# Two heads per keys-times-values matmul in a chunked recurrence with two feed-forward blocks, fp32, one core

## The reference, cut to what matters

```python
# q, k, v, o_gate: [4, 8, 768, 40]; i_gate, f_gate: [4, 8, 768]
for t in range(S):
    m_new = max(f[t] + m, i[t])
    f_stab, i_stab = exp(f[t] + m - m_new), exp(i[t] - m_new);  m = m_new
    C = f_stab * C + i_stab * outer(v[t], k[t])          # 40 x 40 state per head
    n = f_stab * n + i_stab * k[t]
    y[t] = sigmoid(o[t]) * (C @ q[t]) / max(abs(n . q[t]), 1)
x  = y.reshape(3072, 320)
x1 = ((x @ w1) * (x @ w2)) @ w3 @ w_out                   # 320 -> 1024 -> 1024 -> 320
y  = max(x1 @ u1, x1 @ u2, x1 @ u3) @ u_out               # 320 -> 768 -> 320
```

## Time and profile before

| | us |
|---|---|
| median of 3 runs | 710.59 (709.71 to 710.85) |
| profiled execution | 705.52 |
| its span | 703.6 |
| PE busy | 687.3 (98%) |
| PE weight loads busy | 574.5 (82%) |
| DVE busy | 448.6 (64%) |
| ACT busy | 290.5 (41%) |
| POOL busy | 126.1 (18%) |

### The profile page before, as it was taken

The page is one execution under the profiler, slowest core; times in us unless marked ns, Lnnn a source line. Parts: engine busy times, 40 slices in busy tenths (PEclk is TensorE's granted clock), DMA queues, the critical chain, the costliest instruction groups (busy, mean ns, idle before and its releaser), DMA issues.

```text
span 703.6 us, 11573 instructions
## 1 busy us (share of the span) xinstructions
PE 687.3 (98%) x3662; PEld 574.5 (82%) x3662; DVE 448.6 (64%) x819; ACT 290.5 (41%) x640; POOL 126.1 (18%) x153
## 2 busy tenths in 40 slices
PE   5999999999999999999999999999999999999997
PEld 4886888788888888888888888888888888888785
DVE  6678898854688853687853588863578873322423
ACT  1645756333645322654422555422645522322211
POOL 4232434000334100232200143200133200000000
PEclk9999999999999999999999999999999999999999
DMA  8897376060454400355400244510154100100001
GB/s 274 276 270 200 114 202 168 27 146 21 129 134 116 119 25 0 99 140 135 118 24 0 89 122 121 152 33 0 50 153 117 58 0 0 37 1 1 0 1 37
DMA packets 69311, 65.27 MB, mean 93 GB/s; under 512 B 29972, under 2 KB 47700, under 8 KB 69284
## 3 DMA queue, kind: packets, MB, share of 16 engines
q1 hardware_dynamic: 69284, 64.92, 33.3%
HBM read 58.72 MB, written 4.03 MB: 89 GB/s over the span
## 4 chain that ended last, share of the span: by engine, by line
PE 88%; DVE 3%; DMA 3%; issue 2%; SPq 1%; ACT 1%; POOL 0%; POOLq 0%
PE ring L448 52%; PE acc L448 22%; PE ybank L448 9%; PE sbank L448 3%; DMA og_s<-in_og 3%; PE tbank L448 1%; PE tbank L535 1%; DMA w1o_raw<-in_wout 1%; DVE gate L890 1%; ACT gm L655 1%; DVE sc_s L841 0%; DVE hid L911 0%; DVE q_st L851 0%; POOL decay_s L409 0%; DVE x1T L1009 0%
## 5 line engine op out<-in xcount | busy, mean ns | idle before, releaser
L448 PE MATMUL ring<-x1T,mx_hi 128*128 128x512 f32 x432 | 152.5, 393 | 0.1
L448 PE MATMUL ring<-xT,ab_hi 128*128 128x512 f32 x384 | 136.6, 396 | 0.0
L655 ACT ACTIVATE gm<-hid 128x512 fp32r<-128x512 f32 x84 | 53.1, 632 | 164.9 <-DVE hid L923 131.2
L409 POOL TENSOR_TENSOR decay_s<-decay_s,causal 128x512 f32<-128x512 f32 x48 | 63.2, 1317 | 205.3 <-DMA og_s<-in_og 197.9
L448 PE MATMUL acc<-gm,wp 128*128 128x512 f32 x384 | 97.4, 395 | 0.4 <-DVE gm L904 0.4
L448 PEld LDWEIGHTS ring<-x1T,mx_hi 128*128 128x128 f32 x432 | 81.2, 188 | 17.6 <-issue 0.5
L904 DVE TENSOR_TENSOR gm<-hid,gm 128x512 fp32r<-128x512 f32 x84 | 58.2, 692 | 54.2 <-ACT gm L655 54.2
L655 ACT ACTIVATE left<-ring 128x512 f32<-128x512 f32 x84 | 49.9, 594 | 87.5 <-PE ring L448 87.5
L448 PEld LDWEIGHTS acc<-gm,wp 128*128 128x128 f32 x384 | 71.6, 188 | 16.9 <-ACT gm L655 0.8
L448 PE MATMUL ring<-x1T,mx_lo 128*128 128x512 f32 x216 | 84.1, 389 | 0.0
L448 PEld LDWEIGHTS ring<-xT,ab_hi 128*128 128x128 f32 x384 | 72.2, 188 | 14.4 <-ACT xT L655 0.2
(11 more groups left out here) (130 smaller groups left out, 1020.0 us busy)
## 6 DMA issues: line engine op xcount, KB each, us to landing
decay_s<-phi_d SPq DMA_DIRECT2D x48, 256.0 KB
k_s<-in_kT SPq DMA_DIRECT2D x40, 240.0 KB
q_s<-in_qT SPq DMA_DIRECT2D x40, 240.0 KB
w_raw<-in_w3T SPq DMA_DIRECT2D x8, 512.0 KB, 4.5
kn_s<-in_kn SPq DMA_DIRECT2D x48, 80.0 KB
og_s<-in_og SPq DMA_DIRECT2D x48, 80.0 KB
vn_s<-in_vn SPq DMA_DIRECT2D x48, 80.0 KB, 2.4
out_y<-stage SPq DMA_DIRECT2D x12, 256.0 KB, 2.1
```

Source lines behind the costliest of these rows:

```text
L409: pool.tensor_tensor(d4, d4, causal[:].unsqueeze(1).broadcast_to([P, HQ, L]), ALU.add).then_inc(s["masked"], 1)
L448: return pe.matmul(o, l, r, start=start, stop=stop)
L655: return act.activation(o, i, ACT.Copy)
```

## The change

The keys-times-values product of a quad is done in two matmuls, one for each pair of heads: 80 stationary columns (`kw_s` of both heads) and 84 moving ones (`vn_s` of both heads). Of the 80 x 84 result only the two blocks on the diagonal mean something: rows 0 to 39 with the first head's 42 columns, rows 40 to 79 with the second's. The state takes this layout, `state[80, side, quad, pair, 42]`, the blocks off the diagonal included, and `ybank` is written so that a side's pairs lie together. VectorE fades and adds in one scalar_tensor_tensor for each pair, with a factor for each of the 80 rows. These factors are the exponentials of the chunk-end sums, all made once: the sums go out to `last_d` and come back to `last_s` over 40 rows twice (two small loads), ScalarE makes `fades`, and VectorE copies a chunk's 16 columns to `fade_now` and the `since` factors to `since_now` once in each body (`chunk_factors`). GpSimd's fades and ScalarE's small exponentials go.

High and low parts of the state are written to `c_part` (over xT's memory; for chunk 0 `c_first`, over x1T's), and six DMAs of 40 rows bring the diagonal blocks to `c_st`. For the last chunk there is no keys-times-values product, no weighing of keys, no load of `kn_s`, no fade and no stacking; so body 4 is written out too, and the loop covers bodies 1 to 3. Two orders shift: the pieces of `beside1` behind its fourth place go one iteration earlier, and weight piece 6 is loaded behind quad 7 of the opening, not ahead of it.

```diff
             def stack_state(c):
                 sp.wait_ge(s["c_lo"], c + 1)
-                sp.dma_start(c_st[DIM:2 * DIM].bitcast(F32), state[LOW:LOW + DIM]).then_inc(s["c_in"], 16)
-                sp.dma_start(c_st[2 * DIM:ST].bitcast(F32), c_st[0:DIM].bitcast(F32)).then_inc(s["c_in"], 16)
+                parts = c_parts(c)
+                for r, part in enumerate((0, 1, 0)):
+                    for side in range(2):
+                        sp.dma_start(f32(c_st[r * DIM:(r + 1) * DIM, side]).rearrange("p k j d -> p (k j d)"),
+                                     f32(parts[side * DIM:(side + 1) * DIM, part, side * (CW // 2):(side + 1) * (CW // 2)])
+                                     ).then_inc(s["c_in"], 16)
...
-                load_piece(k)
-            load_piece(QUADS)
+                    sp.dma_start(last_d, g_phi[:].rearrange("b (c t) -> b c t", t=L)[:, :, L - 1],
+                                 allow_slow_non_contiguous=True).then_inc(s["last_out"], 16)
+                if k == 4:
+                    sp.wait_ge(s["last_out"], 16)
+                    for side in range(2):
+                        sp.dma_start(last_s[side * DIM:(side + 1) * DIM],
+                                     last_d.rearrange("(j s) c -> s j c", s=2)[side].partition_broadcast(DIM)
+                                     ).then_inc(s["fades_in"], 16)
+                if k < N_AB:
+                    load_piece(k)
+            for n in range(N_AB, N_AB + NSTAGE):
+                load_piece(n)
...
                 for h in range(HQ):
                     hs, hd = slice(h * L, (h + 1) * L), slice(h * DN, (h + 1) * DN)
-                    mm(ybank[:, hd], sc_s[:, slot, hs], vn_s[:, slot, h, :], True, True)
+                    last = mm(ybank[:, hd], sc_s[:, slot, hs], vn_s[:, slot, h, :], True, True)
                     if not first:
-                        mm(ybank[:, HQ * DN + h * DN:HQ * DN + (h + 1) * DN], q_st[:, slot, hs], c_st[:, k, hd], True, True)
-                    last = mm(ybank[0:SQ, 2 * HQ * DN + h * DN:2 * HQ * DN + (h + 1) * DN],
-                              kw_s[:, slot, h * DIM:h * DIM + SQ], vn_s[:, slot, h, :], True, True)
+                        last = mm(ybank[:, HQ * DN + h * DN:HQ * DN + (h + 1) * DN], q_st[:, slot, hs],
+                                  c_st[:, h % 2, k, h // 2, :], True, True)
+                if not final(c):
+                    for j in range(PAIRS):
+                        last = mm(across(ybank[0:PAIR, 2 * HQ * DN:3 * HQ * DN])[:, :, j, :],
+                                  kw_s[:, slot, j * PAIR:(j + 1) * PAIR], vn_s[:, slot, 2 * j:2 * j + 2, :], True, True)
...
             def x_hi(c, u):
                 act.wait_ge(s["turned"], 3 * c + u + 1)
+                if u == 0 and not (isinstance(c, int) and c in (0, CHUNKS - 1)):
+                    act.wait_ge(s["c_in"], 16 * C_LOADS * (c + 1))
...
-                dve.wait_ge(s["faded_ok"], n - QUADS + 1)
-                dve.tensor_tensor(state[0:DIM, k, :], ybank[0:DIM, 2 * HQ * DN:3 * HQ * DN], faded[:, slot, :], ALU.add)
+                if not final(c):
+                    for j in range(PAIRS):
+                        mine = state[:, :, k, j, :]
+                        dve.scalar_tensor_tensor(out=mine, in0=mine, scalar=fade_now[:, k * PAIRS + j:k * PAIRS + j + 1],
+                                                 in1=across(ybank[0:PAIR, 2 * HQ * DN:3 * HQ * DN])[:, :, j, :],
+                                                 op0=ALU.mult, op1=ALU.add)
...
-        beside1 = [[], [N_AB, N_AB + 1], [N_AB + 2], [N_AB + 3], [], [N_AB + 4], [N_AB + 5], [N_AB + 6]]
+        beside1 = [[], [N_AB, N_AB + 1], [N_AB + 2], [N_AB + 3], [N_AB + 4], [N_AB + 5], [N_AB + 6], []]
```

More of the change, by code:

```diff
@@ L103, in build @@
         sc_s = sb("sc_s", [P, 2, HQ * L])
[L104 to L108, removed]
+        kw_s = sb("kw_s", [P, 2, HQ * DIM])
+        state = sb("state", [PAIR, 2, QUADS, PAIRS, DN])
+        c_st = sb("c_st", [ST, 2, QUADS, PAIRS, DN], F32R)
+        last_s = sb("last_s", [PAIR, QUADS * PAIRS, CHUNKS])
+        fades = sb("fades", [PAIR, CHUNKS, QUADS * PAIRS])
+        fade_now = sb("fade_now", [PAIR, QUADS * PAIRS])
+        since_now = sb("since_now", [P, BH])
         heads = sb("heads", [P, HQ, DN])
@@ L222, in quad, with final, quad_loaded, c_parts @@
             return c * QUADS + k
+        def final(c):
+            return isinstance(c, int) and c == CHUNKS - 1
+        def quad_loaded(c, k):
+            if final(c):
+                return 16 * (LOADS * c * (QUADS // 2) + (LOADS - 1) * (k // 2 + 1))
+            return 16 * LOADS * (c * (QUADS // 2) + k // 2 + 1)
+        def c_parts(c):
+            return c_first if isinstance(c, int) and c == 0 else c_part
+        def across(pairs):
+            return pairs.rearrange("p (s j d) -> p s j d", j=PAIRS, d=DN)
         def split(n):
@@ L368, in _ @@
             body(0, False)
-            with sp.Fori(1, CHUNKS - 1) as c:
+            with sp.Fori(1, CHUNKS - 2) as c:
                 body(c, True)
+            body(CHUNKS - 2, True)
             store_group(CHUNKS - 2)
@@ L414, in weigh_keys @@
                 w4 = gcol[:, c, 2 * BH + k * HQ:2 * BH + (k + 1) * HQ].unsqueeze(2).broadcast_to([P, HQ, DIM])
-                pool.tensor_tensor(kw_s[:, slot, 0:HQ * DIM].rearrange("p (h e) -> p h e", e=DIM),
+                pool.tensor_tensor(kw_s[:, slot, :].rearrange("p (h e) -> p h e", e=DIM),
                                    kn_s[:, slot, :].rearrange("p (h e) -> p h e", e=DIM), w4, ALU.mult).then_inc(s["kw_ok"], 1)
[L418 to L430, removed]
-                    fade_state(c, k)
-                    if k + 1 < QUADS:
-                        mask(c, k + 1)
-                        weigh_keys(c, k + 1)
             pool.wait_ge(s["gcol_ok"], 2)
@@ L440, in _ @@
             pool.wait_ge(s["gcol_rest"], 2)
-            with pool.Fori(1, CHUNKS) as c:
-                body(c)
+            with pool.Fori(1, CHUNKS - 1) as c:
+                for k in range(QUADS):
+                    mask(c, k)
+                    weigh_keys(c, k)
+            for k in range(QUADS):
+                mask(CHUNKS - 1, k)
         @block.tensor
@@ L646, in _ @@
             body(0, True)
-            with pe.Fori(1, CHUNKS - 1) as c:
+            with pe.Fori(1, CHUNKS - 2) as c:
                 body(c, True)
+            body(CHUNKS - 2, True)
             body(CHUNKS - 1, False)
@@ L700, in c_hi @@
                 act.wait_ge(s["evacuated"], QUADS * (c + 1))
-                copy(c_st[0:DIM], state[0:DIM]).then_inc(s["c_hi"], 1)
+                copy(c_parts(c)[:, 0, :], state[:].rearrange("p s k j d -> p (s k j d)")).then_inc(s["c_hi"], 1)
             def y_dup(c):
@@ L742, in first_out @@
                 wait(act, s["y_ok"], k)
-                copy(state[0:DIM, k, :], ybank[0:DIM, 2 * HQ * DN:3 * HQ * DN])
+                copy(state[:, :, k, :, :], across(ybank[0:PAIR, 2 * HQ * DN:3 * HQ * DN]))
                 copy(heads[:], ybank[:, 0:HQ * DN].rearrange("p (h d) -> p h d", d=DN)).then_inc(s["evacuated"], 1)
@@ L791, in body @@
                             piece_hi(n)
-                    if more and j == 0:
+                    if more and j == 0 and not final(c + 1):
                         c_hi(c + 1)
@@ L804, in _ @@
             body(0, True)
-            with act.Fori(1, CHUNKS - 1) as c:
+            with act.Fori(1, CHUNKS - 2) as c:
                 body(c, True)
+            body(CHUNKS - 2, True)
             body(CHUNKS - 1, False)
@@ L991, in body @@
                     hidden_mult(c, i)
+                    if more and i == 0:
+                        chunk_factors(c + 1)
                     if more and i >= 2:
@@ L1020, in body @@
                         gate_out(c + 1, QUADS - 1)
-                        c_lo(c + 1)
+                        if not final(c + 1):
+                            c_lo(c + 1)
                     if isinstance(c, int) and c == 0:
@@ L1033, in _ @@
             body(0, True)
-            with dve.Fori(1, CHUNKS - 1) as c:
+            with dve.Fori(1, CHUNKS - 2) as c:
                 body(c, True)
+            body(CHUNKS - 2, True)
             body(CHUNKS - 1, False)
```

70 lines of the change are left out of this document (42 added, 28 removed).

## The result

The changed kernel takes 705.07 us (median of 13 runs, 701.82 to 709.54), the kernel before in the same rounds 710.59 (13 runs): ratio 0.9932, interval 0.9906 to 0.9957, 3 to 7 us less. The forecast was 701.3 us, 9.3 less; 705.07 lies at the slow edge of the stated range (697.8 to 705.4). The profiled executions: 702.67 us against 705.52, spans of 700.6 and 703.6. What was worked out for the chunk bodies came, with something on top of it; the way to block 2 of body 0, which was to gain 0.9 us, lost 6.4. Two executions of all that follow, one of e2_write (756.76 us) and one of e15_best (1176.12 us), ran at a far lower granted clock than the rest (0.85 and 0.62), and the ratios leave them out.

A forecast was written before the change was run, and what follows sets the result against it. TensorE, busy 98% of the span, was taken as the bound. Bodies 1 to 3 4.6, body 4 3.8, body 0 -0.3, opening 1.2 sum to 9.3 us off 710.59: 701.3 us, range 697.8 to 705.4.

The forecast's parts named there:

- What was worked out for the chunk bodies: Block 1: 0.19 us less a quad, 4.6 us over bodies 1 to 3; 3.8 us in body 4 without kw_s.
- the way to block 2 of body 0: Opening plus block 1 of body 0: 1.2 us gained in the opening, 0.3 us lost in body 0.
- three small transfers: Opening, ahead of quads 3 and 5: chunk-end sums out and back, 0.5 to 0.6 us of issue each, while SyncE waits anyway.
- The rest of the opening: Opening: weight piece moved behind quad 7 lands that quad up to 2 us earlier; with shorter attends, 1.2 us taken (0 to 3.3).
- next late: Opening, before attend 7: once quad 7 lands earlier, VectorE itself, with gate work until 0.98 us before its weigh.
- The pair pass: Keys-times-values matmul of two heads: 72 ns a pass from loading 80 columns (bounds 60 and 112), 0.19 us less a quad.
- starts above 80 ns: Sign that the prediction is wrong: pair matmul records in ybank starting more than 80 ns apart, where 72 was expected.
- VectorE in the bodies: Block 1, bodies 1 to 4: new state form 0.24 us each, 0.1 us more a quad, covered by VectorE's free time.
- the wait of about 3 us of TensorE for VectorE: End of body 0's block 1: expected sign that TensorE still waits about 3 us for VectorE.
- 9 us free. Cost nothing: Stacking: six copies end near 258 us, ScalarE's first xT copy runs at 266.95; for chunk 0 some 2 to 3 us free.
- The rival with this mechanism: Stacked copies come too late for xT's first copy in block 2 of four bodies: 4.7 us slower, 715.3 us; chance 0.02.
- the rule on exclusion: Body 0: two-input VectorE and GpSimd SBUF instructions exclude each other; without fades, 1 to 2 us more gained by the rule.

The follow-up runs named there:

- e2_write: e1_onchip with the 192-packet, 4-byte write of chunk-end gates into DRAM put back, read by nobody; 705.8 us, ratio 0.9955.
- e15_best: e6_stack_first again with more runs: changed kernel, fades made on the chip, state copies ahead of the next chunk's quads; 698.8 us, ratio 0.9839.
- e1_onchip: Changed kernel with the fades brought to 80 rows on the chip, without the DRAM write and two broadcast reads, same addresses; 698.55 us, ratio 0.9842.
- e6_stack_first: e1_onchip with the six stacked-state copies issued ahead of the next chunk's first quad in every body but the first; 698.85 us, ratio 0.9846.
- e7_keep_last: e1_onchip with the last chunk's keys loaded, weighed and multiplied and its state updated as in other chunks; 698.73 us, ratio 0.9859.
- e8_moved_back: e1_onchip with 624 unused bytes ahead of stage, so the late tiles lie where the kernel before has them; 700.8 us, ratio 0.9902.
- e12_gm_back: e1_onchip with 640 unused bytes ahead of gm alone, so gm, hid and left lie as in the kernel before; 700.0 us, ratio 0.9904.
- e10: e2_write with the gates first packed by VectorE, so the write is 32 packets of 24 bytes; 694.56 us, ratio 0.983.
- e11: e2_write with its 192 packets of 4 bytes written 512 bytes apart in DRAM; 697.98 us, ratio 0.9853.

## Why the prediction was wrong

**The failed step** is the one of the opening: "three small transfers (...) at 0.5 to 0.6 us of issue each, in places where SyncE then waits for an attend anyway". I priced them by their issue and asked whether SyncE had time. (Even the issue was off: 0.68 us for the write and 4.94 for the two reads.) What they cost is the time of the transfers behind them. To block 2 of body 0 (opening and body 0's block 1), the mean is 132.96 us for the four profiles with the instructions of before, 131.28 for the six with the fades made on the chip and no such transfer (e1, e6, e7, e8, e12, e15), and 140.2 for the changed kernel's two: 8.9 us for three transfers of 31 KB together.

Up to there TensorE is idle for 15.8 us in the changed kernel's two profiles and 11.1 in the six, and its granted clock is at 0.50 for 13.8 us and for 4.0 in the mean. At half the clock a busy stretch loses up to half of its length, so about half of the 8.9 us is the waits and half the clock behind them (an estimate from these figures).

The Trainium skill has the rule that I should have weighed ("DMA: Bandwidth & Descriptors", rules for kernel authors): a strided last dimension becomes one descriptor for each element; the trace agrees: the write has 192 elements, and from 24 to 26 us the changed kernel has 231 packets of 4 bytes, e1_onchip 24. The Trainium skill also says there ("DMA: Bandwidth & Descriptors", specifications) that transfers under 512 bytes are read, modified and written; that holds for e2, e10 and e11 alike and doesn't tell the dear one from the two that cost nothing measurable.

**The rest of the opening** failed too, though its sum looks right. Without the transfers the way to block 2 is 1.7 us shorter where I had 0.9, on profiles that spread by 6 us. But the step was that moving a weight piece behind quad 7 lets that quad land up to 2 us earlier (mask near 53.5) and takes TensorE's wait ahead of attend 7 away. In e1_onchip, GpSimd's mask of quad 7 and TensorE's attend 7 are:

```profile
56.10 1.39 POOL L448 TENSOR_TENSOR decay_s<-decay_s,causal 128x512 f32<-128x512 f32 x1 [3.32 <-DMA og_s<-in_og]
...
60.69 1.72 PE L481 MATMUL ybank<-vn_s,sc_s 128*128 128x42 f32 x8 [1.94 <-DVE sc_s L882]
```

In the six profiles without the transfers the mask starts at 54.6 to 56.9 us and the wait is 1.5 to 2.1 us; in the four of before it is 55.4 to 56.7 and 1.6 to 1.9. To block 2 TensorE is idle for 11.1 us in both groups. In five of the six VectorE goes into that `weigh` without idle time, so it and not the load ends last, as the prediction named for "next late". Where the 1.7 us come from, if they are more than spread, stays open.

**The pair pass** was right: 72 ns from the load of 80 columns; four records take 289 ns, 72 each (in each attend of bodies 1 to 3 one gap is 115 or 116 ns and the last 28 or 29, so "starts above 80 ns" was the wrong sign to look for). With the tiles where before has them (e8_moved_back), block 1 of body 2 takes 60.77 us, 62.16 before: 1.39 us for the forecast 1.5. Body 4 takes 58.37, 62.16 before: 3.79 for 3.8.

**VectorE in the bodies** 1 to 4 was covered, as said. The new form lasts 290 ns, not 240; TensorE's waits for VectorE there come to 0.5 us in all. In body 0 the wait of about 3 us of TensorE for VectorE did not come: before the last attend it is 0.8 us in the changed kernel and 1.1 in e1_onchip. Block 1 of body 0 takes 61.8 and 67.3 us in the changed kernel's two profiles and 64.3 to 67.0 in the four of before, so what VectorE cost there isn't settled.

**Body 0 and the stacked copies.** "9 us free. Cost nothing" held in bodies 1 to 3, read from body 1, and failed in body 0: there SyncE is busy with weight pieces until 153 us, the copies went out at 160.10 and ScalarE waited 3.49 us for them. Block 2 of body 0 took 46.63 us for 45.57: 1.06 us, once. Against 45.35 in e6_stack_first and e15_best, whose tiles lie as the changed kernel's, it is 1.3. The rival with this mechanism had the right place and the wrong body. What the rule on exclusion that the prediction cites from the Trainium skill ("SBUF — State Buffer", who interferes with whom) would have given, a body 0 shorter by the fades, stays open: q_st and k_st together last 13.5 us in body 0 before, and 11.7, 12.1 and 13.6 in the changed kernel, e1_onchip and e15_best, none of which has the fades.

**What no step had** is the place of `gm`. Tiles that shrank by 640 bytes moved it, and some 3 us came free. Without this luck the changed kernel would have been about 2 to 3 us under before and not 5.

The sum over the profiled executions: forecast 9.3, less 7.3 up to block 2 of body 0, less 1.1 for the stacking in body 0, and some 3 more for the addresses: 3.9, where the spans differ by 3.0.

## What to carry to other kernels

Price a transfer in a full queue by what stands behind it, not by its bytes or its issue: look at the packets that it makes, and take small data over partitions with a small matmul when TensorE passes by anyway (0.55 us here). Read the slack of a moved step in every body that differs, the first above all. When tiles change size, compare the instructions that the change doesn't touch too, and give the tiles back their addresses before judging the change.

## What was not expected of the hardware

- 192 writes of 4 bytes side by side into 768 bytes of DRAM took 9.6 us and held 4096-byte packets of other transfers for up to 4.1 us; 512 bytes apart, or as 32 of 24 bytes, 3.8 to 4.3 us and no harm (e10, e11).
- The start of `gm`, `hid` and `left` in SBUF sets how far apart 512-column fp32r matmuls start: 228 ns with gm at byte 213120, 234 to 235 at 213152, 234 at 213760 and 213792. The 512-column matmuls of the same kernels that don't read gm change by about 1 ns. Which of the three tiles it is, and what is special about 213120, wasn't tried.
- Behind a wait of 2.7 us the granted clock stayed at 0.50 for 6.83 us; in the kernel before, behind 1.6 us, it did for 3.41. The length of the wait doesn't set it: behind the wait ahead of attend 7 the clock was at 0.50 for 6.83 us in e1_onchip (1.94 us), for 3.41 in e12_gm_back (2.09 us) and not at all in e7_keep_last (1.94 us) and e15_best (2.04 us). Such stretches are part of the spread of runs of one kernel.
